# Masked copies moved in front, an fp32 first layer and fewer low weights in the prologue of an attention and MoE kernel

## The chip, the cores and the metric

The kernel runs on one core of a Trainium2 chip. Its metric is the device time in microseconds (us) of one execution. The engines are TensorE (PE; its weight loads are PEld), VectorE (DVE), ScalarE (ACT), GpSimd (POOL), and SyncE (SP), whose queue issues every DMA here.

## The reference

A gated linear attention (4 sequences of 768 tokens, 8 heads of 48) is followed by a mixture of 4 experts and a second layer with a hard-swish gate, over 3072 tokens of 384 features:

```
state = alpha[t] * state + outer(k[t], v[t]);  y[t] = q[t] @ state
p = domain_probs / (sum(domain_probs) + 1e-9)
x = sum over e of p[:, e] * (relu(y @ w1[e]) @ w2[e])        # 4 x (384 -> 1024 -> 384)
h = x @ w_in;  out = (h * clip(h + 3, 0, 6) / 6) @ w_out      # 384 -> 2048 -> 384
```

## The kernel before, in words

Attention goes by 48 chunks of 64 tokens, the layers by 6 tiles of 512 tokens (8 chunks each). The order of work on each engine is written out by hand, and semaphores couple the engines.

For a chunk n, VectorE scales the queries by products of alpha (`scale_q`, 7 steps) and POOL the keys (`decays`, `scale_k`, `decay_all`). TensorE computes `score(n)` in fp32, one block of columns for each level of a binary splitting of the chunk. Of these scores, ScalarE copies the coarse levels into `p_kept` (`copy_high`), and VectorE copies the rest under masks (`keep`: step 0 the diagonal, L765, steps 1 to 3 the fine levels, L779). `attend(n)` (L606, L586, L621) multiplies `p_kept` and the queries with the values and the state. VectorE then updates the state (`next_state`, L832 or L835) and transposes the result (`turn_y`, L841). ScalarE (`x_hi`, L1069) and VectorE (`x_lo`, L847), both called `split_x`, split it into two fp32r parts. `score(n+2)` in the prologue waits for `split_x(n)`, as it overwrites the same banks.

A layer has slots g of 128 hidden features. `weights_hi` (ScalarE, L1094) and `weights_lo` (POOL, L1221) split the slot's weights, loaded raw by `load_w` into a ring of four, in two fp32r parts. `hidden(g)` (L653) sums three fp32r products, hi hi, hi lo and lo hi, for each of 3 blocks of 128 features; `hidden_hi` and `hidden_lo` apply the relu and split again; `project(g)` (L672) is the second layer, two slots behind.

The **prologue** handles chunks 0 to 7 (tile 0). TensorE's order in it: `score(n+1)`, a filler product (`keep_warm`, L629, fp32), `attend(n)`, `turn_k(n+1)`, and, after chunks 4, 5 and 6, two early products each: `hidden` of slots 0 to 5 on the first half (256 columns) of tile 0. The **main loop** then walks 288 slots, with chunks 8 to 47 spread among them. VectorE's order in the prologue is `keep(n)` mixed with scalings of chunk n+2, the `hidden_lo` of early products, `next_state(n)`, `turn_y(n)`, a scaling, `split_x(n)`, the last scaling:

```
for step in range(keeps(n)):
    keep(n, step)
    if step < beside:
        scale_q(ahead, at + step)
```

POOL splits the low weights of slots 0 to 5 in its chunks 3 to 8, between the first key step and the decays.

Of the kernel before, what the change touches and what calls it, by code (L numbers as in the profile page):

```python
# [13 lines left out]
P = 128  # L14
CH = 64
# [9 lines left out]
K3 = 3  # L25
# [17 lines left out]
EARLY = 6  # L43
# [147 lines left out]
def build(nc, qa, kk, v, dp, w, diag, level, ident, prob_scratch, out):  # L191
    TOK = TILES * TILE

    with ExitStack() as ctx:
# [66 lines left out]
        out_last = sem("out_last")  # L261
# [145 lines left out]
        def _(sp):  # L407
# [13 lines left out]
            def load_w(g):  # L421

                need(sp, w_hi_made, g - RAW + 1)
                need(sp, w_lo_made, g - RAW + 1)
                u = PHASE_OF[g]
                f = g - STARTS[u] + (0 if PHASES[u][0] == "E" else E_SLOTS)
                sp.dma_start(w_raw[:, g % RAW, :], w[f]).then_inc(in_w[g % RAW], 16)
# [26 lines left out]
            for n in range(PER_TILE):  # L454
                load_qk(n + QRING)
                if n > 0:
                    load_v(n + 1)
                if RAW <= n < LOAD_AHEAD:
                    load_w(n)
# [7 lines left out]
            for g in range(SLOTS):  # L467
                if g + LOAD_AHEAD < SLOTS:
                    load_w(g + LOAD_AHEAD)
                if g in SCORE_AT and SCORE_AT[g] + QRING < CHUNKS:  # L470
                    load_qk(SCORE_AT[g] + QRING)
                if g in STATE_AT and STATE_AT[g] + 2 < CHUNKS:
                    load_v(STATE_AT[g] + 2)
                if g in PROBS_AT:
                    load_probs(*PROBS_AT[g])
                for t in range(TILES - 1):
                    if g == M_START[t] + M_SLOTS + BEHIND:
                        for k in range(K3):
                            store(t, k)
# [5 lines left out]
        def _(pe):  # L485
# [145 lines left out]
            def hidden(g, early=False):  # L631

                kind, t = PHASES[PHASE_OF[g]]
                first = g == STARTS[PHASE_OF[g]] and not early
                cols = columns_of(g, early)
                if early:
                    pe.wait_ge(x_hi_made, EARLY_FROM)
                    pe.wait_ge(x_lo_made, EARLY_FROM)
# [6 lines left out]
                need(pe, hh_made, made(g, early) - 2)  # L645
                need(pe, hl_made, made(g, early) - 2)
# [36 lines left out]
            for n in range(PER_TILE):  # L683
# [10 lines left out]
                for g in early_after(n):  # L694
                    hidden(g, early=True)
# [15 lines left out]
        def _(dve):  # L711
# [218 lines left out]
            for step in range(3, Q_STEPS):  # L930
                scale_q(1, step)
            for n in range(PER_TILE):
# [4 lines left out]
                if n == PER_TILE - 1:  # L937
                    for step in range(1, keeps(n)):
                        keep(n, step)
                    for step in range(beside):  # L940
                        scale_q(ahead, at + step)
                else:
                    for step in range(keeps(n)):
                        keep(n, step)
                        if step < beside:
                            scale_q(ahead, at + step)
# [7 lines left out]
                turn_y(n)  # L954
                if not last:
                    scale_q(ahead, at + behind)
                if n == PER_TILE - 2:
                    keep(n + 1, 0)
                split_x(n)
                if n == PER_TILE - 1:  # L960
                    next_state(n)
                if not last:
# [39 lines left out]
        def _(act):  # L1002
# [57 lines left out]

            def split_x(n):
# [49 lines left out]
            for n in range(PER_TILE):  # L1111
# [9 lines left out]
                if n < EARLY:  # L1121
                    weights_hi(n)
                split_x(n)
# [4 lines left out]
            for g in range(SLOTS):  # L1128
# [9 lines left out]
                if EARLY <= g + SPLIT_AHEAD < SLOTS:  # L1138
# [15 lines left out]
        def _(pool):  # L1154
# [76 lines left out]
            for n in range(K_BEFORE):  # L1231
                for l in range(K_STEPS):
                    if l < LEVELS - 1 or n >= PER_TILE:
                        scale_k(n, l)
                    if l == 0 and 0 <= n - K_BEFORE + EARLY + 1 < EARLY:
                        weights_lo(n - K_BEFORE + EARLY + 1, 2)
# [3 lines left out]
            for g in range(SLOTS):  # L1240
                if EARLY <= g + SPLIT_AHEAD < SLOTS:
# [71 lines left out]
```

## Time and profile before

| what | value |
|---|---|
| median of 3 runs | 1358.62 us (1358.08 to 1358.93) |
| profiled execution, its own time | 1358.82 us |
| span from first to last instruction in it | 1357.0 us |
| mean granted TensorE clock | 0.995 of full speed |
| busy share of the span: PE, DVE, ACT, POOL | 99%, 53%, 43%, 58% |
| chain that ended last: share on PE | 89% |

The span leaves out 1.8 us around the first and the last instruction. The clock is given as a share of 2.4 GHz. A busy share is a mean over a short prologue and a long main loop, which have different limits.

### The profile page before, as it was taken

What the parts mean: (1) busy time and instruction counts of PE and PEld (TensorE: products, weight loads), DVE (VectorE), ACT (ScalarE), POOL (GpSimd) and SP (SyncE); (2) the same over time, 40 slices, a digit from 0 to 9 for tenths busy, and PEclk for the clock granted to TensorE, in tenths of its full rate; (3) what the DMA queues carried; (4) which work ended last, traced back from release to release, by engine and by line L of the source; (5) the groups of instructions that cost most, each with busy time, mean ns of one, the idle gap of its engine ahead of it and who ended that gap; (6) DMA issues with size and microseconds to landing.
All of it is one profiled execution on the core that took longest, in us unless ns stands there. A gap on an engine that the chain in (4) does not pass through costs nothing.

```text
span 1357.0 us, 32289 instructions
## 1 busy us (share of the span) xinstructions
PE 1336.9 (99%) x12348; PEld 1091.1 (80%) x12348; DVE 724.0 (53%) x1582; ACT 585.1 (43%) x1238; POOL 781.3 (58%) x862
## 2 busy tenths in 40 slices
PE   7899999999999999999999999999999999999999
PEld 5687788888888888888888888888888888888887
DVE  7857765555555555555555555555555433333333
ACT  5643334333454343355433345433335433335543
POOL 8956766566556655656565655656564344444442
PEclk7999999999999999999999999999999999999999
DMA  5343333333333433333433333343332343333331
GB/s 164 114 146 103 118 118 117 107 117 97 108 118 116 131 105 120 99 110 105 151 105 112 104 109 116 108 137 112 95 98 83 101 125 108 106 93 94 101 121 35
DMA packets 76039, 150.27 MB, mean 111 GB/s; under 512 B 8816, under 2 KB 33648, under 8 KB 75888
## 3 DMA queue, kind: packets, MB, share of 16 engines
q1 hardware_dynamic: 75888, 148.21, 35.9%
q8 instruction: 101, 1.65, 0.5%
q14 instruction: 50, 0.41, 0.1%
HBM read 143.41 MB, written 4.77 MB: 109 GB/s over the span
## 4 chain that ended last, share of the span: by engine, by line
PE 89%; ACT 0%; issue 0%; DVE 0%; ACTq 0%; DVEq 0%
PE psum L672 42%; PE psum L653 40%; PE psum L540 2%; PE psum L532 1%; PE psum L586 1%; PE psum L606 1%; PE psum L576 1%; PE psum L621 1%; PE psum L523 1%; DVE psum L861 0%; DVE x_lo L893 0%; ACT gate L1075 0%; DVE result L897 0%; ACT q_parts L1042 0%; ACT h_hi L1087 0%
## 5 line engine op out<-in xcount | busy, mean ns | idle before, releaser
L1221 POOL TENSOR_TENSOR w_lo<-w_raw,w_hi 128x768 fp32r<-128x768 f32 (+1 forms) x294 | 531.9, 1810 | 531.3 <-ACT w_hi L1094 531.2
L1087 ACT ACTIVATE h_hi<-psum 128x512 fp32r<-128x512 f32 (+1 forms) x288 | 170.9, 594 | 587.7 <-DVE psum L855 506.7
L672 PE MATMUL psum<-h_hi,w_hi 128*128 128x512 f32 x855 | 341.4, 399 | 0.2 <-DVE x_lo L893 0.2
L653 PE MATMUL psum<-x_hi,w_hi 128*128 128x512 f32 (+1 forms) x882 | 339.8, 385 | 0.7 <-issue 0.7
L653 PE MATMUL psum<-x_lo,w_hi 128*128 128x512 f32 (+1 forms) x882 | 339.3, 385 | 0.0
L653 PE MATMUL psum<-x_hi,w_lo 128*128 128x512 f32 (+1 forms) x882 | 339.2, 385 | 0.0
L672 PE MATMUL psum<-h_hi,w_lo 128*128 128x512 f32 x855 | 333.6, 390 | 0.0
L672 PE MATMUL psum<-h_lo,w_hi 128*128 128x512 f32 x855 | 333.0, 389 | 0.0
L855 DVE SCALAR_TENSOR_TENSOR psum<-psum,probs 128x512 f32<-128x512 f32 x184 | 128.5, 699 | 315.1 <-PE psum L653 314.8
L1094 ACT ACTIVATE w_hi<-w_raw 128x768 fp32r<-128x768 f32 x288 | 241.5, 838 | 0.2
L873 DVE TENSOR_TENSOR h_lo<-psum,h_hi 128x512 fp32r<-128x512 f32 x280 | 192.9, 689 | 46.5 <-ACT h_hi L1087 46.3
L653 PEld LDWEIGHTS psum<-x_hi,w_hi 128*128 128x128 f32 x882 | 165.7, 188 | 34.4 <-ACT x_hi L1069 0.7
L653 PEld LDWEIGHTS psum<-x_lo,w_hi 128*128 128x128 f32 x882 | 165.7, 188 | 33.4
L653 PEld LDWEIGHTS psum<-x_hi,w_lo 128*128 128x128 f32 x882 | 165.7, 188 | 33.0
L672 PEld LDWEIGHTS psum<-h_hi,w_lo 128*128 128x128 f32 x855 | 160.5, 188 | 34.7
L672 PEld LDWEIGHTS psum<-h_hi,w_hi 128*128 128x128 f32 x855 | 160.5, 188 | 34.0 <-issue 0.6
L672 PEld LDWEIGHTS psum<-h_lo,w_hi 128*128 128x128 f32 x855 | 160.8, 188 | 31.1
L861 DVE SCALAR_TENSOR_TENSOR psum<-gate,psum 128x512 f32<-128x512 f32 x96 | 66.7, 695 | 187.7 <-ACT gate L1075 187.7
L1075 ACT ACTIVATE gate<-psum,three 128x512 f32<-128x512 f32 x96 | 66.3, 690 | 129.9 <-PE psum L653 129.9
L779 DVE COPY_PREDICATED p_kept<-level_sb,psum 128x128 f32<-128x128 int32 x304 | 97.9, 322 | 8.4
L1202 POOL TENSOR_TENSOR k_lev<-k_lev,decay 128x256 f32<-128x256 f32 x144 | 96.5, 670 | 6.5 <-DVE decay L720 0.2
L1165 POOL TENSOR_TENSOR decay<-decay 128x64 f32<-128x64 f32 (+3 forms) x184 | 59.2, 322 | 12.0
(81 smaller groups left out, 964.0 us busy)
## 6 DMA issues: line engine op xcount, KB each, us to landing
w_raw<-w SPq DMA_DIRECT2D x288, 384.0 KB, 3.1
alpha_q<-qa SPq DMA_DIRECT2D x48, 256.0 KB, 3.9
k_raw<-kk SPq DMA_DIRECT2D x48, 128.0 KB, 3.5
probs<-prob_scratch SPq DMA_DIRECT2D x24, 256.0 KB, 3.7
v_sb<-v SPq DMA_DIRECT2D x48, 96.0 KB, 2.8
out<-result SPq DMA_DIRECT2D x18, 256.0 KB, 3.8
level_sb<-level SPq DMA_DIRECT2D x1, 128.0 KB, 3.1
ident_sb<-ident SPq DMA_DIRECT2D x1, 64.0 KB, 2.9
```

What stands on the lines that cost most here:

```text
L653: mm = pe.matmul(h_bank[g % 2][:, cols], a, x[:, cols], start=k == 0 and i == 0, stop=k == K3 - 1 and i == 2)
L672: mm = pe.matmul(out_bank[k], a, x, start=first and i == 0, stop=(last or g == PLAIN - 1) and i == 2, skip_group_check=ph == 0)
L779: dve.copy_predicated(dst.rearrange("p a (m r x) -> p a m r x", r=2, x=x)[:, :, :, 1, :], mask.to_broadcast([P, 4, m, x]), s[:, :, at:at + ...
L855: dve.scalar_tensor_tensor(out=h_bank[g % 2][:, :], in0=h_bank[g % 2][:, :], scalar=0.0, in1=probs[:, t % 2, u, :], op0=ALU.max, op1=ALU.m ...
L861: dve.scalar_tensor_tensor(out=h_bank[g % 2][:, :], in0=gate[:, g % 2, :], scalar=6.0, in1=h_bank[g % 2][:, :], op0=ALU.min, op1=ALU.mult) ...
L873: op = dve.tensor_tensor(lo, h_bank[g % 2][:, :], hi, ALU.subtract)
L1075: act.activation(gate[:, g % 2, :], h_bank[g % 2][:, :], ACT.Relu, bias=three[:, :]).then_inc(gate_made, 1)
L1087: act.activation(h_at(h_hi, x_hi, g)[:, cols], h_bank[g % 2][:, cols], ACT.Relu if g < PLAIN else ACT.Copy).then_inc(hh_made, 1)
L1094: act.activation(w_hi[:, g % RING, :], w_raw[:, g % RAW, :], ACT.Copy).then_inc(w_hi_made, 1)
L1165: pool.tensor_tensor(decay_pair(n, l), first, second, ALU.mult).then_inc(z_made, 1)
L1202: op = pool.tensor_tensor(b, a, dec.to_broadcast([P, m, 2, x]), ALU.mult)
L1221: op = pool.tensor_tensor(w_lo[:, g % RING, cols], w_raw[:, g % RAW, cols], w_hi[:, g % RING, cols].bitcast(F32), ALU.subtract)
```

## The change

In the prologue only, with what this asks of the main loop's first slots:

- VectorE's masked copies of chunk n+1 are issued in iteration n: step 0 right after `turn_y(n)`, steps 1 to 3 after `split_x(n)` and one scaling. Those of chunk 0 stand in front of the loop.
- The early products become `hidden_early`: three fp32 matmuls on the raw weights and on an unsplit copy of the first four chunks' outputs, which ScalarE writes into `result` (`keep_x`, new).
- `weights_hi` in the prologue covers slots 0 to 3 instead of 0 to 5, `weights_lo` slots 0 to 3 in POOL's chunks 5, 6, 8 and 9 instead of slots 0 to 5 in chunks 3 to 8. Slots 4 and 5 are split in slots 1 and 2 of the main loop.
- `load_w` also waits for the early products that read the ring's buffer, and the loads of slots 4 and 5 are issued later.

```diff
-EARLY = 6
+EARLY = 2 * DEEP
+SPLIT_EARLY = 4
+SPLIT_AT = {5: 0, 6: 1, 8: 2, 9: 3}
...
                 need(sp, w_hi_made, g - RAW + 1)
                 need(sp, w_lo_made, g - RAW + 1)
+                need(sp, h_made, min(g - RAW + 1, EARLY))
...
-                if RAW <= n < LOAD_AHEAD:
-                    load_w(n)
+                if RAW < n <= EARLY:
+                    load_w(n - 1)
...
+            def hidden_early(g):
+
+                pe.wait_ge(x_kept_made, EARLY_FROM)
+                need(pe, hh_made, made(g, early=True) - 2)
+                need(pe, hl_made, made(g, early=True) - 2)
+                pe.wait_ge(in_w[g % RAW], 16 * (g // RAW + 1))
+                for k in range(K3):
+                    mm = pe.matmul(h_bank[g % 2][:, 0:HALF], w_raw[:, g % RAW, k * P:(k + 1) * P], result[:, k, 0:HALF],
+                                   start=k == 0, stop=k == K3 - 1)
+                mm.then_inc(h_made, 1)
...
                 for g in early_after(n):
-                    hidden(g, early=True)
+                    hidden_early(g)
...
+            for step in range(keeps(0)):
+                keep(0, step)
             for n in range(PER_TILE):
...
-                if n == PER_TILE - 1:
-                    for step in range(1, keeps(n)):
-                        keep(n, step)
-                    for step in range(beside):
-                        scale_q(ahead, at + step)
-                else:
-                    for step in range(keeps(n)):
-                        keep(n, step)
-                        if step < beside:
-                            scale_q(ahead, at + step)
+                for step in range(beside):
+                    scale_q(ahead, at + step)
...
                 turn_y(n)
+                if n < PER_TILE - 1:
+                    keep(n + 1, 0)
+                split_x(n)
                 if not last:
                     scale_q(ahead, at + behind)
-                if n == PER_TILE - 2:
-                    keep(n + 1, 0)
-                split_x(n)
                 if n == PER_TILE - 1:
                     next_state(n)
+                else:
+                    for step in range(1, keeps(n + 1)):
+                        keep(n + 1, step)
                 if not last:
                     scale_q(ahead, at + behind + 1)
...
+            def keep_x(n):
+
+                act.wait_ge(yt_made, n + 1)
+                cols = slice(n * CH, (n + 1) * CH)
+                act.activation(result[:, :, cols].rearrange("p b (h t) -> p b h t", h=2), y_blocks(n), ACT.Copy
+                               ).then_inc(x_kept_made, 1)
...
-                if n < EARLY:
+                if n < EARLY_FROM:
                     weights_hi(n)
+                    keep_x(n)
                 split_x(n)
...
-                if EARLY <= g + SPLIT_AHEAD < SLOTS:
+                if SPLIT_EARLY <= g + SPLIT_AHEAD < SLOTS:
                     weights_hi(g + SPLIT_AHEAD)
...
-                    if l == 0 and 0 <= n - K_BEFORE + EARLY + 1 < EARLY:
-                        weights_lo(n - K_BEFORE + EARLY + 1, 2)
+                    if l == 0 and n in SPLIT_AT:
+                        weights_lo(SPLIT_AT[n], 2)
...
-                if EARLY <= g + SPLIT_AHEAD < SLOTS:
+                if SPLIT_EARLY <= g + SPLIT_AHEAD < SLOTS:
                     weights_lo(g + SPLIT_AHEAD)
```

## Rows read from the trace of the kernel before

**Rows 1.** Busy time by stretches; columns in the first line, the clock as a share.

```profile
core 0: us, PE busy (x) PEld busy (x) DVE busy (x) ACT busy (x) POOL busy (x), PEclk, DMA share, GB/s
38.22:45.48 7.26, 5.01 (x185) 3.70 (x185) 5.96 (x17) 4.84 (x18) 7.26 (x15) 1.00 0.45 124
64.69:79.20 14.51, 13.35 (x267) 11.66 (x267) 10.86 (x35) 5.72 (x20) 8.13 (x16) 1.00 0.63 193
79.20:1357.00 1277.80, 1272.91 (x10591) 1039.22 (x10589) 659.91 (x1404) 538.79 (x1068) 712.65 (x725) 1.00 0.36 109
10.00:20.00 10.00, 8.25 (x207) 6.56 (x203) 7.14 (x17) 6.56 (x26) 9.89 (x23) 0.50 0.78 257
```

**Rows 2.** Timeline of VectorE: start, duration, instruction, count, idle before and its releaser.

```profile
14.80 0.33 DVE L733 TENSOR_TENSOR alpha_q<-alpha_q 128x128 f32<-128x128 f32 x1
...
38.22 0.35 DVE L835 TENSOR_TENSOR state<-state_decayed,psum 128x192 f32<-128x192 f32 x1 [0.65 <-PE psum L621]
...
39.35 0.36 DVE L847 TENSOR_TENSOR x_lo<-psum,x_hi 128x192 fp32r<-128x192 f32 x1 [0.16 <-ACT x_hi L1069]
...
40.25 0.75 DVE L765 COPY_PREDICATED p_kept<-diag_sb,psum 128x256 f32<-128x256 int32 x1
40.79 1.03 DVE L733 TENSOR_TENSOR alpha_q<-alpha_q 128x128 f32<-128x128 f32 x1
...
43.19 0.28 DVE L779 COPY_PREDICATED p_kept<-level_sb,psum 128x128 f32<-128x128 int32 x1
```

**Rows 3.** Timeline of TensorE: `score` (L514), filler (L629) and `attend` (L606).

```profile
26.91 0.43 PE L514 MATMUL psum<-alpha_q,k_raw 64*64 64x32 f32 x16 [0.65 <-POOL k_lev L1181]
...
36.95 0.40 PE L606 MATMUL psum<-v_sb,p_kept 64*32 64x48 f32 x32 [1.62 <-DVE p_kept L779]
...
40.00 0.43 PE L514 MATMUL psum<-alpha_q,k_raw 64*64 64x32 f32 x16 [0.66 <-DVE q_lev L749]
...
41.80 0.70 PE L629 MATMUL psum<-zeros_sb 128*128 128x256 f32 x2
43.57 0.41 PE L606 MATMUL psum<-v_sb,p_kept 64*32 64x48 f32 x32 [1.07 <-issue]
...
50.59 0.41 PE L606 MATMUL psum<-v_sb,p_kept 64*32 64x48 f32 x32 [0.48 <-issue]
```

**Rows 4.** Timeline of POOL, chunks 4 to 6.

```profile
28.86 0.51 POOL L1165 TENSOR_TENSOR decay<-alpha_q 128x128 f32<-128x128 f32 x1
...
39.24 0.62 POOL L1198 TENSOR_TENSOR k_top<-k_lev,decay 128x256 f32<-128x256 f32 x1
...
40.67 2.00 POOL L1221 TENSOR_TENSOR w_lo<-w_raw,w_hi 128x384 fp32r<-128x384 f32 x2
42.64 0.51 POOL L1165 TENSOR_TENSOR decay<-alpha_q 128x128 f32<-128x128 f32 x1
```

**Rows 5.** TensorE: first and last of 18 matmuls; filler, with min/median/max ns.

```profile
45.53 0.36 PE L653 MATMUL psum<-x_hi,w_hi 128*128 128x256 f32 x1
...
47.65 0.28 PE L653 MATMUL psum<-x_hi,w_lo 128*128 128x256 f32 x1
...
62.76 1.56 PE L629 MATMUL psum<-zeros_sb 128*128 128x256 f32 x6
...
L629 PE MATMUL psum<-zeros_sb x46: 377/483/794, 1.2 to 63.9; 128*128 128x256 f32 x46
```

**Rows 6.** Timeline of ScalarE in chunk 1.

```profile
25.15 0.84 ACT L1094 ACTIVATE w_hi<-w_raw 128x768 fp32r<-128x768 f32 x1
26.02 0.33 ACT L1069 ACTIVATE x_hi<-psum 128x192 fp32r<-128x192 f32 x1
```

**Rows 7.** Timeline: start of the main loop on TensorE, and POOL's first low weights there.

```profile
64.69 0.35 PE L653 MATMUL psum<-x_hi,w_hi 128*128 128x256 f32 x1 [0.37 <-issue]
...
76.86 1.85 POOL L1221 TENSOR_TENSOR w_lo<-w_raw,w_hi 128x768 fp32r<-128x768 f32 x1 [4.69 <-ACT w_hi L1094]
```

**Rows 8.** Timeline of TensorE: the first `score`.

```profile
8.66 0.66 PE L514 MATMUL psum<-alpha_q,k_raw 64*64 64x32 f32 x16 [3.69 <-DVE q_lev L749]
```

More of the change, by code:

```diff
@@ L260, in build @@
         h_made, gate_made, h_out, out_weighed = sem("h_made"), sem("gate_made"), sem("h_out"), sem("out_weighed")
-        out_last = sem("out_last")
+        out_last, x_kept_made = sem("out_last"), sem("x_kept_made")
         hh_made, hl_made = sem("hh_made"), sem("hl_made")
@@ L467, in _ @@
             for g in range(SLOTS):
-                if g + LOAD_AHEAD < SLOTS:
+                if EARLY <= g + LOAD_AHEAD < SLOTS:
                     load_w(g + LOAD_AHEAD)
@@ L629, in keep_warm, with hidden @@
                     pe.matmul(out_bank[2][:, 0:2 * P], zeros_sb[:, 0:P], zeros_sb[:, :], start=True, stop=True)
-            def hidden(g, early=False):
-                kind, t = PHASES[PHASE_OF[g]]
[L634 to L638, printed above, removed]
+            def hidden_early(g):
[7 more added lines that the diff above has]
+                mm.then_inc(h_made, 1)
+            def hidden(g):
+                kind, t = PHASES[PHASE_OF[g]]
+                first = g == STARTS[PHASE_OF[g]]
+                cols = columns_of(g)
                 if first and kind == "E":
@@ L644, in hidden @@
                     pe.wait_ge(out_free, K3 * (PHASES.index(("E", t)) + 1))
-                need(pe, hh_made, made(g, early) - 2)
-                need(pe, hl_made, made(g, early) - 2)
+                pe.wait_ge(hh_made, made(g) - 2)
+                pe.wait_ge(hl_made, made(g) - 2)
                 pe.wait_ge(w_hi_made, g + 1)
```

## The prediction, made before the changed kernel ran

> **What bounds the kernel now.** I read the table of stretches first. From 79.20 us to the end TensorE is busy for 1272.91 of 1277.80 us at full clock, and in 64.69:79.20 for 13.35 of 14.51 [rows 1]. So once the main loop runs, only TensorE's own work counts. The change leaves that work as it is, with the same matmuls in the same slots. What can move is the moment at which the loop starts: `hidden(0)`, whose first matmul issues at 64.69 after 0.37 us idle [rows 7]. Before that, in the prologue of eight chunks, TensorE has gaps (5.01 of 7.26 us busy in 38.22:45.48) while POOL is never idle and VectorE is busy for 5.96 us [rows 1]. The prologue is a loop through four engines, so I then read the timelines of each. I call T(n) the start of chunk n's state update on VectorE, right behind `attend(n)`. T(3) is 38.22 [rows 2], and T(4), where the stretch ends, 45.48.
>
> In that one period: VectorE does state, transpose, one scaling, then `split_x` at 39.35, and only at 40.25 the first masked copy of the *next* chunk, with scalings between the copies; the last copy starts at 43.19 [rows 2]. `attend(4)` starts 0.38 us later, at 43.57, though TensorE had issued the filler in front of it from 41.80 and a filler call takes some 0.47 us [rows 3, 5]. Chunk 3 shows the same, named: 1.62 us idle until VectorE's copy L779 [rows 3]. So in chunks 3 and 4 the masked copies end last in front of `attend`. At the other gate, `score(5)` starts at 40.00, and POOL's last needed key step for it (L1198) ran 39.24 to 39.86 [rows 3, 4]; `split_x` ended at 39.71 [rows 2]. POOL and the split are nearly level there.
>
> **Part 1, the copies move in front.** The copies of chunk n+1 now follow chunk n's transpose: first copy, `split_x`, one scaling, three short copies. By their spacings: 0.27 state, 0.30 transpose, 0.54 first copy (40.25 to 40.79), 0.28 split, about 0.4 scaling: `score(n+2)` may start at T(n)+1.8, against 1.78 now (38.22 to 40.00) [rows 2, 3]. The first copy fills the time in which VectorE and ScalarE hand over, so it costs the split almost nothing. Three copies of 0.2 later, at T(n)+2.4, the next `attend` has its input, instead of T(3)+5.25. TensorE reaches it at T(n)+4.05 at the earliest: 1.8 until `score`, 1.80 for `score` (40.00 to 41.80), 0.45 for the filler. The gate of the copies is gone, and what comes next is TensorE's order and POOL. Queued behind the moved copies are the last scaling (about 1 us later than now) and so POOL's first decay of a later chunk; that is why POOL gains little before chunk 5.
>
> **Part 2, fewer low weights.** `weights_lo` of two halves costs POOL 42.64 - 40.67 = 1.97 us [rows 4]. Six calls (POOL chunks 3 to 8) become four (5, 6, 8, 9). In chunks 3 and 4 they filled a wait for the last scaling of chunk n-3, so I work it through. In chunk 1 ScalarE now ends `split_x` at 26.02 + 0.26 + 0.33 = 26.6 [rows 6]; then VectorE has the split (0.28), a scaling (0.4), three copies (0.65) and the last scaling (0.45) until 28.4, where POOL's decay in chunk 4 can start, instead of at 28.86 [rows 4]. So chunk 4's keys are 0.5 us earlier. Chunk 5 then has `w_lo(0)` in it as now and comes 0.5 earlier too: L1198 ends at 39.35, and `score(5)` starts at 39.5. A second effect: the scaling that meets a `w_lo` takes 1.03 us on VectorE (40.79) against 0.33 undisturbed (14.80) [rows 2]. The Trainium skill, SBUF — State Buffer, "Who interferes with whom", says that a VectorE instruction with two SBUF inputs is fully blocked by a GpSimd one that reads SBUF; the trace agrees, since the long scaling ends at 41.82, just behind the first half of `w_lo` (half of 1.97 after 40.67 is 41.66). With the copies moved, such delays (0.7 us here, two a chunk at most) lie beside `score` and `attend` and cost nothing, unless VectorE's sum, about 6.2 us a period, becomes the bound.
>
> Moved into the main loop: `weights_hi/lo(4)` and `(5)` at slots 1 and 2. POOL idles there for 4.69 us before 76.86 [rows 7]; two calls of 1.85 (76.86's duration) and the key steps behind them end near 80, `w_lo(4)` itself near 72, while `hidden(4)` issues at 79.20. Hidden, by 7 us; the price without that cover would be up to 3.7. SP's `load_w(8)` waits for `w_lo(4)` and goes out near 72; its data is wanted in slot 5, behind `hidden(4)`. Also hidden. In the prologue `load_w(4)` and `(5)` now wait for the early products (`h_made` 1 and 2), issue, by the sums below, at about 45 (`attend(4)` at 41.8, 1.5 for it, 1.4 for one product) and 50, and are read after `attend(6)`, at 57. Loads of chunks 10 and 11 queue behind them and aren't wanted before 80.
>
> **Part 3, fp32 first layer.** Each early half product was 9 fp32r matmuls; the 18 of a pair issue from 45.53 to 47.65, 0.125 each, 2.24 together [rows 5]. Now it is 3 fp32 matmuls. The nearest row is the filler, also fp32, 128x256 on 128x128 weights: with two records for each. Six of them take 1.56 us, and with 0.38 for the last one (the shortest is 377 ns) they stand (1.56 - 0.38)/5 = 0.236 apart [rows 5]. A pair is 12 x 0.236 = 2.83 us: +0.6 a pair, +1.8 to +1.95 for three. Bounds: nothing, if the fp32 records stood as close as 2.24/12 = 0.19, and +2.3 a pair, if they did not overlap at all (12 x 0.38 = 4.5). I take 0.65 by the filler, whose shape, type and weight loads are the same, and keep both ends. The Trainium skill, FP8 and Floating Point Precision, "TensorE Precision Notes", counts four passes for true fp32; by passes, 3 x 4 against 9 is a third more, some +0.75 a pair, so page and filler both speak against this part.
>
> ScalarE loses `weights_hi(4)` and `(5)` and gains four `keep_x`. The nearest is the copy L1069, 0.33 us for the same shape [rows 6]. It stands before `split_x`; in chunk 1, where ScalarE ends its weights at 25.99 and starts the split at 26.02 [rows 6], it pushes `score(3)` from 26.91 [rows 3] to about 27.4. `attend(2)` still comes no later, since its copies, too, no longer stand in front of it.
>
> **The sum**, gain on `attend(n)` as it goes. Chunk 3: 36.95 to 35.2, 1.75. Chunk 4: `score(5)` 39.5 + 1.80 + 0.5 = 41.8, gain 1.8 (POOL caps it). Chunk 5: +0.5, since `attend(5)` too stood behind 0.48 us of idle [rows 3] that the copies explain, -0.65 for fp32: 1.65. Chunk 6, where no such gap is: -0.65, so about 1.0. Chunk 7: -0.65: 0.4. Main start: +0.35, the idle before 64.69 [rows 7], as VectorE no longer comes late to the transpose of chunk 7: 0.75. Two short pauses with no cause shown (0.45 and 0.6 us, inside `attend(4)` and `attend(6)`) may be absorbed or recur; I add 0.15. Gain 0.9 us. The span goes from 1357.0 to 1356.1, the profiled execution from 1358.82 to 1357.9, and the median, 0.20 below the profiled one, from 1358.62 to **1357.7**.
>
> **Rivals.**
> (A) The whole gain shows: POOL lets `score(5)` go at 38.5, both pauses go, fp32 costs half as much. 0.9 + 1.0 + 1.0 + 1.0 = 3.9, 1354.7. For it: four periods of 6.1 to 7.3 us against 5.5 by TensorE's path. Against it: POOL has no idle time to give in 38.22:45.48 [rows 1], and `w_lo(0)`, 1.97 us, stays in chunk 5. 7%.
> (B) The copies' gain is lost because `copy_high` or `keep_x` on ScalarE takes their place as the last input, and fp32 is paid in full: +1.95, 1360.6. For it: in chunk 6 I have `copy_high` ending only 0.1 us before the first copy wants it. 14%.
> (C) The clock, which ends slower. TensorE idled for 3.69 us before `score(0)`, and the stretch 10:20 ran at 0.50 [rows 1, 8], the lower level, 1.2 GHz. The new wait before `score(5)` is about 1.9 us by my sum (0.66 now). If POOL is late enough that it passes about 3.7 us, the clock falls, and one such stretch (some 12 us) costs a pair of fp32 products 2.3 more and `score` and `attend` 1.5 a chunk: +5, 1363. 5%.
> (E) fp32 records that don't overlap, the upper bound: 1357.7 + 3 x 1.65 = 1362.6, with no other mishap; from +1.2 a pair more on it ends slower. Against it: the filler. 2%.
> (D) No effect: the prologue is POOL's after all and both parts cancel within 0.3 us; 1358.6. 20%.
>
> **The numbers.** Forecast 52%. A measurement here can't tell less than 0.2%, 2.7 us, from no change: faster needs 1355.9 or less, slower 1361.3 or more. Forecast, (D) and (B) lie inside. Faster 0.08 (A, and a tail of the forecast), same 0.84, slower 0.08 (C, E, and (B) with more). Range: low 1355.8 (the forecast with both pauses gone and fp32 at half), high 1360.4 (to (B)).
>
> **What would show it.** `attend(3)` at 35.2 and `attend(4)` near 41.9 without VectorE in front; `score(5)` released by POOL near 39.5; pairs of fp32 products 2.8 us long; `hidden(0)` at 63.8; `w_lo` calls near 70 to 76 and no new TensorE idle after 72; clock 1.00 from 25 on. Wrong, if the fp32 records are longer than 0.24 apart, if ScalarE ends last before the copies, or if TensorE stops at `hidden(4)` for weights.

## The result, and the profile after

The changed kernel takes 1365.87 us (median of 6 runs, 1365.11 to 1366.91), the kernel before 1358.78 in the same session (6 runs, 1358.08 to 1360.73): ratio 1.0045, 95% interval 1.0035 to 1.0055. It is slower by 0.45%, some 6 us by the ratio (the two medians are 7.1 us apart), and lies outside the predicted range. The profiled execution took 1366.51 us with a span of 1364.6, against 1357.0.

The loss arises before the main loop. `hidden(0)` now starts at 71.49 us instead of 64.69 [rows 7], 6.8 of the 7.6 us by which the span grew. First the part between the state updates of chunks 1 and 6 as one stretch; columns as in [rows 1]. After:

```profile
26.87:64.90 38.03, 32.29 (x937) 25.11 (x937) 31.66 (x81) 23.87 (x95) 30.06 (x64) 0.82 0.30 89
```

Before, the same instructions:

```profile
25.13:58.81 33.68, 26.69 (x950) 21.47 (x950) 29.67 (x83) 25.17 (x94) 33.68 (x63) 1.00 0.38 108
```

POOL, never idle before, now has 8 us to spare. TensorE's idle time fell only from 7.0 to 5.7 us, and its busy time rose by 5.6. Of this the fp32 products explain about 1; the rest stands beside the clock, 0.82 instead of 1.00.

The timeline of TensorE after, the rows that answer to [rows 3, 5, 7]:

```profile
29.16 0.43 PE L517 MATMUL psum<-alpha_q,k_raw 64*64 64x32 f32 x16 [1.17 <-DVE q_lev L760]
...
31.32 0.40 PE L609 MATMUL psum<-v_sb,p_kept 64*32 64x48 f32 x32
...
33.19 0.37 PE L624 MATMUL psum<-state,q_lev 64*32 64x48 f32 x22 [0.86 <-issue]
...
36.52 0.65 PE L517 MATMUL psum<-alpha_q,k_raw 64*64 64x32 f32 x16 [1.68 <-DVE q_lev L760]
...
40.38 0.57 PE L609 MATMUL psum<-v_sb,p_kept 64*32 64x48 f32 x32
...
44.87 0.65 PE L517 MATMUL psum<-alpha_q,k_raw 64*64 64x32 f32 x16 [0.37 <-DVE q_lev L760]
...
49.11 2.75 PE L641 MATMUL psum<-result,w_raw 128*128 128x256 f32 x12
51.79 0.43 PE L517 MATMUL psum<-alpha_q,k_raw 64*64 64x32 f32 x16
...
55.38 0.41 PE L609 MATMUL psum<-v_sb,p_kept 64*32 64x48 f32 x32 [1.35 <-issue]
...
57.06 4.01 PE L641 MATMUL psum<-result,w_raw 128*128 128x256 f32 x12
...
65.01 2.75 PE L641 MATMUL psum<-result,w_raw 128*128 128x256 f32 x12
...
71.49 0.27 PE L664 MATMUL psum<-x_hi,w_hi 128*128 128x256 f32 x1 [0.76 <-ACT x_hi L1084]
```

`attend` (L609) waits for VectorE nowhere: the copies' gate is gone, as forecast. Three other things took its place: `score` (L517) waits for a scaling (L760), there are pauses for which the trace shows no releaser, and stretches run at the lower clock. The clock by stretches:

```profile
22.00:24.00 2.00, 2.00 (x84) 2.00 (x83) 1.77 (x7) 0.49 (x3) 1.09 (x2) 0.50 0.00 0
24.00:26.00 2.00, 2.00 (x62) 1.30 (x59) 0.72 (x2) 1.18 (x6) 2.00 (x5) 0.64 0.06 13
34.00:36.00 2.00, 0.84 (x5) 0.41 (x3) 1.95 (x5) 1.65 (x8) 2.00 (x6) 0.92 0.19 49
36.00:38.00 2.00, 1.48 (x56) 1.51 (x60) 1.90 (x8) 0.90 (x5) 1.50 (x2) 0.50 0.03 8
44.00:46.00 2.00, 1.63 (x47) 1.16 (x48) 1.90 (x7) 1.42 (x7) 0.36 (x2) 0.52 0.00 1
56.00:58.00 2.00, 2.00 (x49) 1.65 (x42) 1.28 (x4) 0.59 (x3) 2.00 (x5) 0.54 0.28 83
```

Before, it had risen for good by 24. It is the lower level, 1.2 GHz, until about 25.5, from 35.7 to 45.9 and from 56.2 to 59.6 (the share of each row gives the moment). The first fall lies inside the 1.68 us of idle time in front of `score(4)`, the second 0.8 us behind the pause of 1.35.

The late rise at 25.5 isn't a fixed trait of the kernel. Two kernels further down (wide and narrow fillers) are the same up to `attend(1)`; in their profiled executions the clock rose at 22.1 and at 25.5, and T(1) is 25.11 and 26.73, against 26.87 here. From T(1) to the start of the main loop it is 39.56 us before and 44.62 after; that part of the 6.8 us, 5.1, doesn't hang on the rise.

VectorE after, chunk 1 and the scalings that gate chunks 4 and 5:

```profile
26.87 0.35 DVE L846 TENSOR_TENSOR state<-state_decayed,psum 128x192 f32<-128x192 f32 x1 [2.04 <-PE psum L624]
27.14 0.39 DVE L852 STREAM_TRANSPOSE psum<-psum 128x192 f32<-128x192 f32 x1
27.44 0.71 DVE L776 COPY_PREDICATED p_kept<-diag_sb,psum 128x256 f32<-128x256 int32 x1
28.22 0.36 DVE L858 TENSOR_TENSOR x_lo<-psum,x_hi 128x192 fp32r<-128x192 f32 x1
28.49 0.42 DVE L760 TENSOR_TENSOR q_lev<-q_lev,decay 128x256 f32<-128x256 f32 x1
28.82 1.10 DVE L790 COPY_PREDICATED p_kept<-level_sb,psum 128x128 f32<-128x128 int32 x3
...
35.28 0.99 DVE L760 TENSOR_TENSOR q_lev<-q_lev,decay 128x256 f32<-128x256 f32 x1
...
43.79 0.82 DVE L760 TENSOR_TENSOR q_lev<-q_lev,decay 128x256 f32<-128x256 f32 x1
```

From T(1) = 26.87 to `score(3)` at 29.16 are 2.29 us, and 2.87 and 2.70 in the next two chunks, against 1.78 to 1.88 before. The scaling of 0.42 takes 0.99 and 0.82 where it meets `weights_lo` on POOL:

```profile
35.00 2.13 POOL L1237 TENSOR_TENSOR w_lo<-w_raw,w_hi 128x384 fp32r<-128x384 f32 x2
...
45.97 0.45 POOL L1181 TENSOR_TENSOR decay<-alpha_q 128x128 f32<-128x128 f32 x1 [1.64 <-DVE q_lev L760]
...
76.67 1.82 POOL L1237 TENSOR_TENSOR w_lo<-w_raw,w_hi 128x768 fp32r<-128x768 f32 x1 [5.40 <-ACT w_hi L1109]
```

ScalarE in chunk 1:

```profile
27.56 0.33 ACT L1073 ACTIVATE result<-psum 128x192 f32<-128x192 f32 x1 [0.26 <-DVE psum L852]
27.79 0.33 ACT L1084 ACTIVATE x_hi<-psum 128x192 fp32r<-128x192 f32 x1
```

The waits of VectorE from 19 to 64 (us in total, times, longest): the two engines wait in turn, VectorE 5.7 us for `attend`, TensorE 1.17, 1.68 and 0.37 for a scaling in the same stretch.

```profile
DVE state L846 <- PE psum L624: 5.7, 4, 2.0
```

Chunk by chunk, T(n) (start of the state update on VectorE; for chunk 7 its transpose), and what the rows show behind each difference:

| n | T before | T after | period before, after | what lies behind it |
|---|---|---|---|---|
| 0 | 18.97 | 19.25 | | |
| 1 | 25.13 | 26.87 | 6.16, 7.62 | `score(2)` 0.56 later, lower clock to 25.5 instead of 22.2 |
| 2 | 31.22 | 33.65 | 6.09, 6.78 | T to `score` 2.29, pause 0.86 |
| 3 | 38.22 | 42.17 | 7.00, 8.52 | T to `score` 2.87, lower clock |
| 4 | 45.48 | 49.21 | 7.26, 7.04 | T to `score` 2.70, half of it at the lower clock |
| 5 | 52.05 | 56.72 | 6.57, 7.51 | pause 1.35, fp32 pair +0.5 |
| 6 | 58.81 | 64.90 | 6.76, 8.18 | pair of 4.01 at the lower clock, pause 0.27 |
| 7 | 63.39 | 69.96 | 4.58, 5.06 | fp32 pair |

### The profile page after: what moved, and what is told of

It reads as the page before. It is cut to its first block, busy times and chain, and to the rows that moved or that the text cites. A ratio compares the mean times of both kernels' runs of the same rounds, so it can differ in the third digit from the quotient of the medians.

```text
span 1364.6 us, 32249 instructions
## 1 busy us (share of the span) xinstructions
PE 1344.2 (99%) x12330; PEld 1096.1 (80%) x12330; DVE 730.4 (54%) x1582; ACT 585.6 (43%) x1242; POOL 779.2 (57%) x860
## 3 DMA queue, kind: packets, MB, share of 16 engines
q8 instruction: 101, 1.65, 0.5%
## 4 chain that ended last, share of the span: by engine, by line
PE 88%; ACT 0%; issue 0%; DVE 0%; DVEq 0%; ACTq 0%
PE psum L683 41%; PE psum L664 40%; PE psum L543 2%; PE psum L535 1%; PE psum L589 1%; PE psum L609 1%; PE psum L579 1%; PE psum L624 1%; PE psum L526 1%; DVE psum L872 0%; DVE x_lo L904 0%; ACT gate L1090 0%; DVE result L908 0%; ACT h_hi L1102 0%; ACT x_hi L1116 0%
## 5 line engine op out<-in xcount | busy, mean ns | idle before, releaser
L664 PE MATMUL psum<-x_hi,w_hi 128*128 128x512 f32 (+1 forms) x864 | 334.4, 387 | 1.1 <-ACT x_hi L1084 0.8
L664 PE MATMUL psum<-x_lo,w_hi 128*128 128x512 f32 (+1 forms) x864 | 334.2, 387 | 0.0
L664 PE MATMUL psum<-x_hi,w_lo 128*128 128x512 f32 (+1 forms) x864 | 334.1, 387 | 0.0
L664 PEld LDWEIGHTS psum<-x_hi,w_hi 128*128 128x128 f32 x864 | 162.2, 188 | 34.5 <-ACT x_hi L1084 0.9
L664 PEld LDWEIGHTS psum<-x_lo,w_hi 128*128 128x128 f32 x864 | 162.2, 188 | 33.4
L664 PEld LDWEIGHTS psum<-x_hi,w_lo 128*128 128x128 f32 x864 | 162.2, 188 | 33.0
```

The lines of the kernel that those rows point to most:

```text
L664: mm = pe.matmul(h_bank[g % 2][:, cols], a, x[:, cols], start=k == 0 and i == 0, stop=k == K3 - 1 and i == 2)
```

## The experiments

Each was timed in several rounds against the kernel before on the same chip; ratios are against that kernel, with 95% intervals. "Main start" is the start of `hidden(0)` in the profiled execution (64.69 before, 71.49 after). It is one execution and can lie off the median: by +2.1 us for the copies alone, by -2.8 for the moved low weights, by -1.9 for the scaling in front. The changed kernel stands at 1.0045, 1.0035 to 1.0055.

### Which part costs

The changed kernel with VectorE's order of before:

```diff
-                for step in range(beside):
-                    scale_q(ahead, at + step)
...
+                    for step in range(keeps(n)):
+                        keep(n, step)
+                        if step < beside:
+                            scale_q(ahead, at + step)
...
                 turn_y(n)
-                if n < PER_TILE - 1:
+                if not last:
+                    scale_q(ahead, at + behind)
+                if n == PER_TILE - 2:
                     keep(n + 1, 0)
                 split_x(n)
-                if not last:
-                    scale_q(ahead, at + behind)
...
-                else:
-                    for step in range(1, keeps(n + 1)):
-                        keep(n + 1, step)
```

> The changed kernel with the masked copies in the order of before: fp32 early products, copies for them and fewer low weights alone. Rival P: most of the loss is here, 1362 to 1366. Theory T (the new order starts the idle before score that lets the clock fall): the clock is 1.00 from 22 on and only fp32's price shows, up to +2, 1357.5 to 1361.

Measured: 1360.29, ratio 1.0005 (0.9996 to 1.0014), main start 64.50. Its TensorE:

```profile
36.68 0.40 PE L609 MATMUL psum<-v_sb,p_kept 64*32 64x48 f32 x32 [1.60 <-DVE p_kept L790]
...
43.58 0.41 PE L609 MATMUL psum<-v_sb,p_kept 64*32 64x48 f32 x32 [1.45 <-issue]
44.91 2.76 PE L641 MATMUL psum<-result,w_raw 128*128 128x256 f32 x12
```

`attend(3)` and `attend(4)` stand where they stood in [rows 3], each 0.10 us behind the last copy, and the clock is low only to 22. So without the new order of the copies there is no loss that can be measured. The fp32 products, `keep_x` and the fewer low weights together cost 0.7 us in the old order, with an interval from -0.5 to 1.9.

The kernel before with the new order of the copies alone (the diff above, reversed, on it):

> The kernel before with the new order of masked copies alone (fp32r early products, six low weights in the prologue as before). Theory T: POOL has no wait in chunks 3 and 4 to lose, the gate of the copies is gone; if the clock stays up, 1355 to 1358; if the later scalings before score (0.5 to 1 us a chunk) leave TensorE idle, the clock falls here too, 1361 to 1366. Rival P (my prediction's part 1 was right, the other parts cost): 1356 to 1357.5, clock 1.00 from 22 on.

Measured: 1362.59, 1.0020 (1.0009 to 1.0030), main start 70.35. The order alone ends slower, by 2.7 us; with the rest of the change beside it, the loss is 6.1. In its profiled execution T(n) to `score` is 2.41, 2.92 and 2.69 us in chunks 1 to 3, though it has no `keep_x`: the order makes this way longer, not the new copy on ScalarE. The two parts by themselves (2.7 and 0.7) make 3.4 of the 6.1 us. The parts aren't additive, then, though the difference is only just clear of the noise.

### The wait in front of `score`

The changed kernel with the copies last, so that `score` waits again for `split_x` alone; then the same order on the kernel before:

```diff
                 turn_y(n)
-                if n < PER_TILE - 1:
-                    keep(n + 1, 0)
+                if not last:
+                    scale_q(ahead, at + behind)
                 split_x(n)
                 if not last:
-                    scale_q(ahead, at + behind)
+                    scale_q(ahead, at + behind + 1)
...
-                    for step in range(1, keeps(n + 1)):
+                    for step in range(keeps(n + 1)):
                         keep(n + 1, step)
-                if not last:
-                    scale_q(ahead, at + behind + 1)
```

> The changed kernel with VectorE's order behind the transpose: scaling, split_x, last scaling, then all four masked copies of the next chunk. Theory S (TensorE is the chain once the copies no longer gate attend, and the changed order made the way from the state update to score longer, 2.3 to 2.9 us instead of 1.8, since first copy, split and scaling stand in series): that way is 1.8 to 2.1 again and the time falls by 3 to 5 us, to 1361 to 1363. Rival C (pauses of TensorE without a releaser and the lower clock make the loss, wherever the order puts them): below 1.5 us of gain, 1364.5 to 1366.

> The kernel before with this same order alone (scaling, split_x, last scaling, then the four copies of the next chunk). Theory S: attend no longer waits for the copies and score isn't later than before, so it is faster than the kernel before by 1 to 3 us, 1356 to 1358.5 on the scale of 1359. Rival C: TensorE's pauses and a low clock take the gain back, 1359 to 1363, as with the copies alone in the changed order (+2.7).

Measured: 1363.22, 1.0021 (1.0011 to 1.0030), main start 68.12; and 1362.86, 1.0017 (1.0008 to 1.0027), 68.71. T(n) to `score` is 1.80, 2.06 and 1.79 us again in chunks 1 to 3 of the first. Taking the first copy and the scaling out from in front of `score` brings back about half of the loss (3.3 us, 1.4 to 5.1). The gain over the kernel before that theory S gave the second did not come. In this second kernel VectorE itself has become the bound. Its stretch between the state updates, with VectorE busy for 34.56 of 36.37 us, and one scaling in it:

```profile
26.04:62.41 36.37, 29.49 (x947) 23.80 (x947) 34.56 (x83) 23.90 (x93) 34.31 (x66) 0.86 0.34 96
```

And from its timeline:

```profile
42.17 0.82 DVE L749 TENSOR_TENSOR q_lev<-q_lev,decay 128x128 f32<-128x128 f32 x1
```

What is missing lies in gaps too short for the view: no row of VectorE there has an idle time in front of it. Scalings of 0.28 to 0.45 us take 0.8 to 1.1 beside POOL's tensor operations, and its mean period is 7.3 us.

The last scaling in front of the short copies (is it POOL's later start that costs?), and the low weights in other chunks (does the collision?), both on the changed kernel:

```diff
                 split_x(n)
                 if not last:
                     scale_q(ahead, at + behind)
+                    scale_q(ahead, at + behind + 1)
...
-                if not last:
-                    scale_q(ahead, at + behind + 1)
...
-SPLIT_AT = {5: 0, 6: 1, 8: 2, 9: 3}
+SPLIT_AT = {3: 0, 4: 1, 7: 2, 8: 3}
```

> The changed kernel with the last scaling in front of copies 1 to 3, the first copy still in front of split_x. Rival K (the last scaling starts POOL's decays, POOL waits 11.7 us in all for it, and its keys gate score): the time falls by 2 us or more. Theory S: POOL's wait is covered, TensorE's score is not released by POOL in any chunk of the changed kernel, so the time stays within 1 us.

> The changed kernel with the four low weights of the prologue in POOL's chunks 3, 4, 7 and 8 instead of 5, 6, 8 and 9, into the waits of 3.7 and 2.6 us that POOL has in chunks 3 and 4. Theory S: the two scalings in front of score that now meet a low weight (0.99 and 0.82 us instead of 0.42, at 35.28 and 43.79) are met in other chunks; the sum of collisions stays, within 1 us of the changed kernel. Rival K (POOL's keys gate score in chunks 5 and 6): score(5) and score(6) come 2 us earlier and the time falls by 2 or more.

Measured: the first 1365.31, 1.0034 (1.0022 to 1.0045), main start 68.30; the second 1364.43, 1.0031 (1.0020 to 1.0042), main start 66.51. In the changed kernel POOL's decays wait 11.7 us for the last scaling in six waits (1.64 in the row above), yet POOL releases no `score`. Giving POOL this scaling earlier moves the time by 1.5 us and moving the collisions by 1.9, both with intervals that overlap that of the changed kernel. Neither is the cause alone. The profiled execution of the second kernel took 1361.65 us, and its clock stayed up from 21.5 on: with the new order and no later low spell, the main start still comes 1.8 us behind that of the kernel before. Its ten runs lie between that and 1366.86.

### The clock

TensorE made colder or warmer by its fillers. On the kernel before, the fillers around chunks 1 and 2 taken out:

```diff
-                    keep_warm(1 if n + 1 < PER_TILE else 3)
+                    keep_warm((0 if n in (1, 2) else 1) if n + 1 < PER_TILE else 3)
...
-                        keep_warm(1)
+                        keep_warm(1 if n in (0, 3) else 0)
```

> The kernel before with the fillers behind attend and behind turn_k of chunks 1 and 2 left out (four filler products). Theory T: with less TensorE work between 25 and 40 us the clock falls there as in the changed kernel, and this alone costs 3 to 6 us, 1362 to 1365. Rival R: even if the clock falls, attend(3) and attend(4) wait for VectorE's copies anyway (1.6 and 1.1 us idle), so a fall costs under 1.5 us, 1358.6 to 1360.

Measured: 1361.37, 1.0004 (0.9994 to 1.0013), main start 67.00. The clock was low from 27.4 to 30.8 and from 34.2 to 41.0 in the profiled execution, whose main start lies 2.3 us behind 64.69. The median shows no loss, with 1.8 us as the upper end; that the other runs had the same low spells isn't shown, and the edit takes work out of TensorE as well. On the changed kernel, more fillers behind `turn_k`; fillers of 512 columns instead of 256 in chunks 1 and 2 (and one in 3); fillers of 32 columns in chunks 1 and 2:

```diff
-                        keep_warm(1)
+                        keep_warm((2, 3, 3, 2)[n])
...
-                    keep_warm(1 if n + 1 < PER_TILE else 3)
+                    keep_warm(1 if n + 1 < PER_TILE else 3, 4 * P if n in (1, 2) else 2 * P)
...
-                        keep_warm(1)
+                        keep_warm(1, 4 * P if n in (1, 2, 3) else 2 * P)
...
-                    keep_warm(1 if n + 1 < PER_TILE else 3)
+                    keep_warm(1 if n + 1 < PER_TILE else 3, 32 if n in (1, 2) else 2 * P)
...
-                        keep_warm(1)
+                        keep_warm(1, 32 if n in (1, 2) else 2 * P)
```

> The changed kernel with one, two, two and one more filler products behind turn_k of chunks 1 to 4, where TensorE idles 0.49, 1.17, 1.68 and 0.37 us before score. Theory T (the loss is the TensorE clock: it rises at 25 instead of 22 us and falls at 36 and at 56): the fall at 36 does not come, the clock is 1.00 from 26 to at least 50, and the time drops by 3 to 6 us, to 1360 to 1363. Rival R (the loss is the chain last scaling to POOL to score, the clock only follows): the fillers lie in idle time or delay score by some tenths, the clock may stay up, and the time stays within 1.5 us of 1365.9.

> The changed kernel with the fillers in chunks 1 and 2 (behind attend and turn_k) and behind turn_k of chunk 3 twice as wide, 512 columns instead of 256, with the number of TensorE instructions kept. They lie in TensorE's idle time before score (1.17 and 1.68 us). Theory K (the lower clock from 35 and from 56 us costs 3 to 5 us): the clock stays up through 35 to 45, score(4) to attend(3) takes 2.2 us instead of 3.9, and the time falls by 2 us or more. Theory F (where the clock stays up, TensorE reaches the next code load sooner and pauses there for it, some 2.2 us behind the load): pauses without a releaser take the clock's place, and the time stays within 1.5 us.

> The changed kernel with the fillers in chunks 1 and 2 (behind attend and turn_k) 32 columns wide instead of 256, the number of instructions kept. TensorE is busy for some 1.5 us less between 27 and 36 us. Theory K: the clock falls earlier or longer there, and the time rises by 1 to 4 us. Theory F: low clock and pauses replace each other, within 1.5 us.

Measured: more fillers 1367.22, 1.0055 (1.0040 to 1.0070), where I expected a gain if the clock was the cause. They cut the spell of 10 us to 3.4, but shift `score`, and pauses of 2.06 and 2.01 us appear. Wide fillers: 1364.31, 1.0035 (1.0023 to 1.0047), main start 68.64, and no low spell after 22 us. Narrow ones: 1366.61, 1.0045 (1.0030 to 1.0060), main start 70.63, with the clock low to 25.5 and from 28.9 to 49.3. So some 24 us more at half the clock stand beside 2.3 us between the medians (4 runs against 8), and the intervals overlap: the price is small against the length, and not clear of zero. In the profiled executions the two take 43.53 (wide) and 43.90 us from T(1) to the main start. What the wide fillers have in place of the clock:

```profile
32.12 0.37 PE L624 MATMUL psum<-state,q_lev 64*32 64x48 f32 x22 [1.13 <-issue]
...
35.19 0.43 PE L517 MATMUL psum<-alpha_q,k_raw 64*64 64x32 f32 x16 [0.57 <-DVE q_lev L763]
...
38.77 0.41 PE L609 MATMUL psum<-v_sb,p_kept 64*32 64x48 f32 x32 [1.34 <-issue]
...
46.60 0.31 PE L624 MATMUL psum<-state,q_lev 64*32 64x48 f32 x12 [0.80 <-issue]
...
53.70 0.41 PE L609 MATMUL psum<-v_sb,p_kept 64*32 64x48 f32 x32 [1.66 <-issue]
```

With 0.29 at 61.16 these pauses sum to 5.2 us, where narrow fillers have one of 0.41. `attend(3)` comes 3.58 us behind `score` here at full clock, and 3.86 in the changed kernel at the lower one.

Last, an attempt to have the clock up earlier in the kernel before, by 11 fillers instead of 4 in front of `score(0)`:

> The kernel before with 11 filler products in front of score(0) instead of 4, into 3.7 us of idle there. If the clock stays up from there on (it is at half from 8.6 to 22.3 us), score(0), score(1) and attend(0) run at 0.6 of their time; VectorE, POOL and ScalarE then set the pace, so of some 4 us of TensorE time 1 to 3 reach the start of the main loop: 1356.5 to 1358.5 on the scale of 1359.3. If the clock falls anyway in the idle at 12 us: no change, or slower by the filler's overhang, up to 0.5.

Measured: 1360.39, 0.9999 (0.9988 to 1.0010). Nothing is gained, but the edit did not do what it was for: the clock fell at 12.5 all the same and rose at 22.7, as late as before. What an earlier rise would be worth stays open.

### What the pauses are

In the packed trace one 16 KB transfer of the queue for instructions stands in front of each of them. The page of DMA queues of the changed kernel for 52 to 56, with the pause that ends at 55.38:

```profile
q1 hardware_dynamic: 427, 0.62, 45.9%
q8 instruction: 1, 0.02, 1.4%
```

Each pause that is named here ended 2.2 to 2.7 us behind the start of one: at 53.1 in the changed kernel and 55.38; at 29.8, 36.2, 43.9, 51.3 and 58.9 with wide fillers, and 32.12, 38.77, 46.60, 53.70 and 61.16. That the pause at 55.38 is no wait for another engine shows in the weight loads (PEld): the first one of `attend(5)` runs at 53.95, the other 31 from 55.38 on.

"issue" alone doesn't tell such a pause, though. In the kernel before, `attend(2)`, `attend(4)` and `attend(5)` start 0.10 us behind the end of VectorE's last copy, whatever the trace names; no transfer stands 2.2 to 2.7 us in front of any of them. They waited for the copies. `attend(3)`, where it names VectorE, is the exception: the last copy ended at 36.57, 0.38 us before it, and a transfer at 34.5 puts the end of a pause at 36.7 to 37.2.

```profile
36.29 0.28 DVE L779 COPY_PREDICATED p_kept<-level_sb,psum 128x128 f32<-128x128 int32 x1
...
50.20 0.28 DVE L779 COPY_PREDICATED p_kept<-level_sb,psum 128x128 f32<-128x128 int32 x1
```

If the pauses hang on the place in the instruction stream, extra instructions must move them. One-column fillers in front of `score(0)`, 16 or 24 of them, and 16 on the wide-filler kernel:

```diff
             keep_warm(4)
+            keep_warm(16, 1)
             score(0)
```

> The kernel before with the same 16 one-column products in front of score(0), done before score(0) can start (24 of them were not). Theory F: the pauses inside attend(4) (45.10) and attend(6) (58.01) move to other instructions; since other places are less well covered than these, the time rises by up to 3 us, or falls by up to 1. Rival: pauses in the same places, time within 0.7 us.

> The kernel before with 24 one-column products in front of score(0), in idle time: some 96 more TensorE instructions, so that every later code load comes that much earlier in the order of work. Theory F: the pauses without a releaser (0.45 us at 44.7, 0.64 at 57.4 in the kernel before) move to other instructions and change size, each still ending about 2.2 us behind a load; the time changes by up to 2 us either way. If the pauses belong to something else (a wait, a bank), they stay where they are and the time stays within 0.5 us.

> The run with wide fillers (clock up from 22 us on, pauses of 0.82 to 1.66 us inside attend(2), before attend(3), inside attend(4), before attend(5)), with 16 one-column products more in front of score(0), in idle time: TensorE's stream is 64 instructions longer there. Theory F (a pause ends about 2.2 us behind a code load, and loads come at fixed places of the stream): each pause moves to an earlier instruction or disappears behind a wait; the sum of the pauses, 5.2 us, changes by more than 1 us and the time with it. Rival (the pauses belong to the work at those places): same places, same sizes, the time within 0.7 us.

Measured: 16 on the kernel before 1360.67, 1.0000 (0.9990 to 1.0010). The pauses moved. The one inside `attend(4)` stood behind 32, 16 and 20 products of `attend`; with the 16 fillers it stands behind 32 and 4, so 32 products earlier:

```profile
45.10 0.31 PE L621 MATMUL psum<-state,q_lev 64*32 64x48 f32 x12 [0.45 <-issue]
```

```profile
44.50 0.43 PE L586 MATMUL psum<-v_sb,k_rows 64*64 64x48 f32 x12 [0.41 <-issue]
```

That is the count of what was added, since each filler has two records. One of 0.48 us stands inside `score` at 40.66, and the one at 58.01 now lies in front of `attend(6)`, at 57.72. `attend(3)`, free of its pause, starts at 36.56, 0.10 us behind the last copy. The total did not change.

The run with 24 gave 1366.83, 1.0034 (1.0018 to 1.0050), but tells nothing of pauses: its fillers took 8.41 us, and `score(0)` came at 11.82 instead of 8.66. The third, 1364.95, 1.0037 (1.0021 to 1.0053), says little of the time: in its profiled execution (1368.92) `score(0)` came at 11.51, and a low spell from 48.1 to 54.9 stands in it. But it shows the same shift by 32 at both places that can be compared. The pause of 1.13 with wide fillers stood behind 32, 16 and 10 products of `attend(2)`, that of 0.29 behind 32, 16 and 11 of `attend(6)`:

```profile
34.53 0.38 PE L609 MATMUL psum<-v_sb,p_kept 64*32 64x48 f32 x26
35.65 0.28 PE L609 MATMUL psum<-v_sb,p_kept 64*32 64x48 f32 x6 [0.73 <-issue]
...
64.47 0.38 PE L609 MATMUL psum<-v_sb,p_kept 64*32 64x48 f32 x27
66.16 0.28 PE L609 MATMUL psum<-v_sb,p_kept 64*32 64x48 f32 x5 [1.30 <-issue]
```

### Is the fp32 work on the chain?

The changed kernel with 2 of the 3 blocks of 128 features in `hidden_early`. It leaves out the third block of features for the first half of tile 0 in slots 0 to 5.

```diff
-                for k in range(K3):
+                for k in range(K3 - 1):
...
-                                   start=k == 0, stop=k == K3 - 1)
+                                   start=k == 0, stop=k == K3 - 2)
```

> The changed kernel with two of the three blocks of each early fp32 product (it leaves out the third block of features of the first layer for the first half of tile 0 in slots 0 to 5), 0.94 us less TensorE work in each of three pairs. Theory S (in the new order TensorE is the chain through the pairs): 2 to 2.8 us faster than the changed kernel. Rival: other engines or code loads fill the gap, under 1 us.

Measured: 1363.76, 1.0022 (1.0013 to 1.0032), 3.1 us less than the changed kernel by the ratios. Its pairs of products:

```profile
47.31 1.89 PE L641 MATMUL psum<-result,w_raw 128*128 128x256 f32 x8
...
62.23 1.89 PE L641 MATMUL psum<-result,w_raw 128*128 128x256 f32 x8
```

At 1.89 instead of 2.75 us a pair (and 3.48 for 4.01 in the one at the lower clock) it saves 2.3 us in these rows, 2.6 if all ran at full clock. The 3.1 us of the ratios are more than this, but their interval goes from 1.3 to 5.0: work on TensorE is on the chain in the new order, to the amount of half of it or all. The profiled executions speak for half. The main start comes 3.0 us earlier, but 2.0 of them are there at T(1) already (24.83 against 26.87, in front of the first pair, where this execution had its clock up earlier); from T(4) to the main start the two differ by 1.2 us (21.11 and 22.28).

## Why the prediction was wrong

**The step that failed** is in part 1: "`score(n+2)` may start at T(n)+1.8", with "The gate of the copies is gone, and what comes next is TensorE's order and POOL". Both halves failed.

- T(n) to `score`: measured 2.29 undisturbed. The first copy takes 0.78 until the split (27.44 to 28.22; it ends at 28.15 and ScalarE's part at 28.12, so the two are level), not the 0.54 that I had read from the start of the next instruction in [rows 2], where a scaling overlapped the copy; and I ended the scaling at its duration, while `score` starts 0.25 behind its end. That is 0.49 together. Where the scaling meets `w_lo`, another 0.4 to 0.6. I had those collisions "beside `score` and `attend`"; with the new order one of them is the last input of `score`. The order test (copies last) shows what the whole of it is worth: 3.3 us (1.4 to 5.1), about half of the loss.
- "Gate gone": the copies no longer wait, and still `attend(3)` at full clock comes 3.58 us behind `score` (wide fillers), against 3.85 before (33.10 to 36.95). The next wait was level with the one removed: a pause in TensorE's instruction supply. I took `attend(3)` for the named example of the copies' gate, but its copies had ended 0.38 us before it, and the pause ended last there. At `attend(4)` my reading of the copies was right, and there a pause of 0.80 stands inside `attend(4)` with wide fillers; in front of `attend(5)` there is one of 1.35 (1.66 with wide fillers), where the copies' wait had been 0.48. With the copies last, VectorE's own sum takes the place of the gate in the kernel before. I saw "two short pauses with no cause shown" and added 0.15 us for them; with wide fillers, at full clock, they sum to 5.2 us in the new order.
- The clock, rival C, was given 5% on the condition of an idle time of 3.7 us. It fell inside an idle time of 1.68 and behind one of 1.35. In the profile it costs much (pair 4.01 instead of 2.75, `score` to `attend` 3.86 instead of 2.16), but some 24 us more of it stand beside only 2.3 us between the medians (narrow and wide fillers, not clear of noise), and the pauses that stand at full clock (5.2 us) are nearly missing at the lower one (0.41).

**Right:** POOL no longer in front of `score(3)`, and a push of it by `keep_x`, though smaller than my 0.5: T(1) to `score(3)` is 2.05 in the old order with `keep_x` against 1.78; a pair of fp32 products 2.75 us against my 2.83; `w_lo(4)` in the main loop at 76.67, hidden; no stop at `hidden(4)`; POOL's first decays queued behind the last scaling. The cost of fp32, three times 0.5 against my 0.65, was nearly right in size where the clock is up.

**Wrong beside it:** POOL released no `score`, neither at 39.5 nor elsewhere. I gave 1.65 to 1.8 us of gain to chunks 3 to 5; with the step above at its measured 2.3 to 2.9, no gain is left to set against the fp32 pairs, and the sign turns. Rival B had the price of fp32 with the copies' gain lost (1360.6), but not that the new gate is worse than the old one.

**What stays open:** how the other half of the 6 us divides between clock and pauses. I argue that the one stands in for the other, from the wide and the narrow fillers; no run has neither. The mean clocks of the runs (0.988 to 1.0 in the six of the changed kernel, with spans from 1363.2 to 1365.0) can't divide it, since such a mean can miss the low spell at the start: the wide fillers with 16 products more show 1.00 at 28 us, where the products of `attend(1)` still have the length that they have at the lower level (0.57 instead of 0.40). Open too is why the order with copies last ends 2.5 to 3 us behind the kernel before in the changed kernel, where VectorE is not always busy. An order with `keep_x` behind `split_x` on ScalarE, which would take it from in front of `score`, wasn't tried. No experiment was faster than the kernel before beyond noise.

## What to carry to other kernels

Before moving the work that ends last in front of a step, list every wait that ends within a microsecond of it, and compare the end of the named releaser with the start of the step: 0.10 us in between means that it was the gate, 0.38 that something else was. In chunk 3 here, removing a wait of 1.6 us bought 0.3, since the next was level with it. In a loop through several engines, cost the new last input of each gate by start to start between rows that are not overlapped, plus the time from its end to the release (0.25 us for a scaling here), and with its collision where it can meet one. Extra work that is free under a wait (fp32 products and the rest in the old order: 1.0005) is paid for once that wait is gone (3.1 us back, 1.3 to 5.0, for 2.3 to 2.6 of work).

## What the runs showed of the hardware

- TensorE pauses 0.3 to 2.1 us at places that hang on its instruction stream, each ending 2.2 to 2.7 us behind the start of a 16 KB transfer of the instruction queue. Sixteen added products of two records each moved three of them by just 32 records. At the lower clock they nearly vanish: 5.2 us in five pauses at full clock against 0.41 in one with long low spells. Not each transfer has a pause behind it.
- The clock fell to the lower level inside an idle time of 1.68 us, and 0.8 us behind one of 1.35; TensorE was busy for 0.84 of 2 us in 34:36, around the first fall. Idle times of this length do not always bring it: with wide fillers 1.34 and 1.66 us passed without a fall.
- VectorE's scalings of 0.28 to 0.45 us took 0.8 to 1.1 us beside POOL's tensor operations, and 0.42 became 0.99 beside `w_lo`.
